# Attention and two networks on one core: one program instead of two, and another order of work where they meet

## Chip, core and metric

The kernel runs on one core of one Trainium2 chip. The metric is the time on the device in microseconds (us). Engines are named as in the profile: PE (TensorE, with PEld for its weight loads), DVE (VectorE), ACT (ScalarE), POOL (GpSimd) and SP (SyncE, which only issues transfers here).

## What is computed

Three stages, each feeding the next. First an attention over chunks of 32 tokens, then a network with a rational activation, then a network with a product of two projections:

```python
# attention: 4 batches, 8 heads, 768 tokens, 64 per head; 8 memory keys; 16 tokens left and 8 right of a chunk of 32
scores = scale * np.matmul(q_c, k_full.transpose(0, 1, 3, 2))
a = np.exp(scores - max); a = a / (sum(a) + 1e-09)
out[:, :, c_start:c_end] = np.matmul(a, v_full)
# x: 3072 tokens of 512
h = x @ w_in                                   # 512 -> 2048
g = (a0 + a1*h + a2*h^2 + a3*h^3) / (1 + |b0|*|h| + |b1|*h^2 + 1e-6)
x2 = g @ w_out                                 # 2048 -> 512
y = ((x2 @ w1) * (x2 @ w2)) @ w3 @ w_out2      # 512 -> 1024 -> 1024 -> 512
```

## The kernel before

**Precision.** Every matrix product of the networks is made of three products on PE, of a high and a low part: hi by hi, hi by lo, lo by hi. The high part is a copy to the type that PE multiplies, the low part is the difference. So a product of a 512x128 piece of weights with 512 tokens is 12 matmuls of 128x128 by 128x512. DVE, ACT and POOL make the parts.

**Two programs in a row.** `attention_and_weights` (L213) opens a block with a program for each engine, and so does `mlps` (L812, block at L856). All engines meet between the two blocks; the trace shows the meeting as L215. The first program folds w3 and w_out2 into one matrix, runs the attention tile by tile (24 tiles t = 0 to 23 of 128 tokens, 6 for a batch, `tile_step` on each engine), and splits the weights of the first network into parts. The second runs both networks over 6 blocks of 512 tokens.

**A tile of attention.** For tile t PE does `transpose_p` (L736: the probabilities are transposed, 8 matmuls), `scores` of tile t+3 (L716) and `pv` (L744). DVE does in one step (L630) the maximum of tile t+1, the sum of t, the subtraction of the maximum of t+1, and the division of t (`normalise`, L616). ACT does (L534) `copy_pT` of t, `exp` of t+2, `copy_xT` of t (from bank 6) and the issue of its store, `store_x`. Each engine works through its queue in order. In this text T(t), norm(t) and pv(t) are those steps of tile t. SP loads v for tile t+3 and one raw piece of w_in or w_out in its step t (L394).

**Weights of the first network.** There are 16 slots, one for each piece of 128 hidden units; a slot has four parts (w_in hi, lo, w_out hi, lo). POOL splits two raw pieces for a slot (`split_weights`, L176: a multiplication by ones for hi, L181, and a subtraction for lo, L184). Slots 0 to 13 are split during the first program; slots 14 and 15 lie where v and the transposed probabilities are kept, and so are split at the start of the second (4 pieces, L947 and the loop behind it).

**The join.** The first block of x is loaded back from the scratch tensor xT by SP at its step 15 (L413), together with the coefficients of the activation (L414, L416). ACT makes x_hi in tiles 18 and 19, two chunks each, behind the tile's other work (L529). DVE makes x_lo of chunks 0 and 2 behind its steps 19 and 20 (L668), POOL those of chunks 1 and 3 behind its last piece (L453). PE puts the products h of slot 0 and 1 with the first block into the two last tiles (L757). Bank 7 is the one in which q and k are turned; from tile 18 on it is free.

**The first network.** For slot m of block i, PE makes h(m) (`h_product`, L205) and, three slots later in its order, adds g(m) times w_out (`finish_g`, L1175, its matmuls at L1183). Between them ACT does `start_h` (|h|, h squared, a linear term; L978, L981, L982), DVE `make_s` (L1082), ACT `ln_exp` (L989, L992, the reciprocal), DVE `make_g` (L1099, L1102, L1106), ACT `g_his` (L997), DVE `make_p` of the next slot (L1089, L1092, which read PSUM) and `make_g_lo` (L1111). I write h(m), f(m) = finish_g of slot m, and g_lo(m), all of the first block unless said. POOL has one more piece of weights of the second network to split after every third g_lo, four in each of the first four blocks (L939, L944), and x_lo of two chunks.

PE's order in a tile of the first program, and its start in the second:

```python
            def tile_step(b, pos, last=False):
                turns = [] if last else [(b + 1, pos // 3, c) for c in TURNS[pos % 3]]
                transpose_p(b, pos)
                for n in turns[0:1]:
                    turn(*n)
                if not last or pos < 3:
                    pe.wait_ge(centred, TPB * b + pos + 2)
                    scores(*after(b, pos, 3))
                elif pos >= TPB - 2:
                    pe.wait_ge(centred, TILES)
                    pe.wait_ge(raw_split, 2 * EARLY + 4)
                    h_product(nc, pe, sh, slot_a, bank, 0, pos - (TPB - 2))
                for n in turns[1:2]:
                    turn(*n)
                pv(b, pos)
...
            start_h(0, 2)
            start_h(0, 3)
            finish_g(0, 0, first=True)
```

Of the kernel before, what the change touches and what calls it, by code (L numbers as in the profile page):

```python
# [79 lines left out]
SM_EPS = 1e-9  # L80
FOLD_TURNS = ((0, 0), (0, 0), (0, 0), (0, 2), (2, 5), (5, 8), (8, 11), (11, 14), (14, 16))
# [17 lines left out]
def build(nc, q, k, v, mem_k, mem_v, w_in, w_out, poly_a, poly_b, w1, w2, w3, w_out2, out,  # L99
          xT, x2T, bweights):  # L100
    with ExitStack() as ctx:
        base = (nc.sbuf_base + 31) // 32 * 32
        end = nc.sbuf_usable_end // 32 * 32

        ctx.enter_context(nc.sbuf_tensor("slab", [P, (end - base) // 4], F32))
        top = end // LINE * LINE
        slots = top - SLOTS * 4 * BLK * 4
        weights = nc.alloc_sbuf_tensor_at("weights", [P, SLOTS * 4 * BLK], F32R, offset=slots)
        work = base
        sh = Shared(nc, ctx, slots, Place(nc, top, end))  # L110
        banks = ctx.enter_context(nc.psum_tensor("banks", [P, 8, 512], F32))
        bank = [banks[:, i, :] for i in range(8)]
        attention_and_weights(nc, q, k, v, mem_k, mem_v, w_in, w_out, w3, w_out2, poly_a, poly_b,
                              xT, bweights, weights, slots, work, banks, bank, sh)
        mlps(nc, w1, w2, w_in, w_out, xT, x2T, bweights, out, weights, work, bank, sh)


class Place:
# [5 lines left out]
    def __call__(self, name, shape, dtype=F32):  # L124
# [6 lines left out]
        return t  # L131


class Shared:


    def __init__(self, nc, ctx, end, tail):
# [17 lines left out]
        self.ln_bias = tail("ln_bias", [P, 2])  # L155
        self.small = tail
# [40 lines left out]
def h_product(nc, pe, sh, slot, bank, i, m, chunks=range(KC)):  # L197


    for c in chunks:  # L200
# [3 lines left out]
        for n, (a, x) in enumerate(((0, sh.x_hi), (0, sh.x_lo), (1, sh.x_hi))):  # L204
            last = nc.tensor.matmul(bank[m % 4][:, :], slot[:, m, a, cols], x[:, c, :],  # L205
# [7 lines left out]
def attention_and_weights(nc, q, k, v, mem_k, mem_v, w_in, w_out, w3, w_out2, poly_a, poly_b,  # L213
                          xT, bweights, weights, base, work, banks, bank, sh):
    with ExitStack() as ctx:  # L215
        x_raw, x_hi, x_lo, coef = sh.x_raw, sh.x_hi, sh.x_lo, sh.coef
        x_loaded, coef_loaded, x_hi_ready = sh.x_loaded, sh.coef_loaded, sh.x_hi_ready
        wf_stored, xt_stored = sh.wf_stored, sh.xt_stored
        raw, raw_loaded, raw_hi_ready, raw_split = sh.raw, sh.raw_loaded, sh.raw_hi_ready, sh.raw_split
        qk_sb = sh.qk_sb  # L220

        def sem(name):
            return ctx.enter_context(nc.semaphore(name))

        def sem2(name):
            return [sem(f"{name}{i}") for i in range(2)]


        fold = Place(nc, base, base + KEPT * 4 * BLK * 4)
        wo2_raw = fold("wo2_raw", [P, JS, DM])  # L230
        wo2_hi = fold("wo2_hi", [P, JS, DM], F32R)
        wo2_lo = fold("wo2_lo", [P, JS, DM], F32R)
        w3_raw = fold("w3_raw", [P, 2, F2])
        w3t_hi = fold("w3t_hi", [P, 2, F2], F32R)
        w3t_lo = fold("w3t_lo", [P, 2, F2], F32R)
        wf = fold("wf", [P, 2, 2, DM], F32R)

        top = Place(nc, base + KEPT * 4 * BLK * 4, base + SLOTS * 4 * BLK * 4)
        v_sb = top("v_sb", [P, V_BUFS, 2, DM])
        pT = top("pT", [P, H, P])  # L240
        memk_sb = pT[0:B * MEM, 0:KC, :].rearrange("p a c -> p (a c)")

        at, small = Place(nc, work, sh.raw_at - 2 * BLK * 4), Place(nc, sh.small.at, sh.small.end)
        ident = small("ident", [P, P])
        ones = small("ones", [P, 1])
        neg_max = small("neg_max", [P, H])
        sums = small("sums", [P, H])
        rsums = small("rsums", [P, H])
        qT = at("qT", [P, 2, PAIRS, HALF])
        kT = at("kT", [P, 2, PAIRS, WINDOWS, KEYS])  # L250
        probs = at("probs", [P, 2, H, KEYS])
        memkT = at("memkT", [P, PAIRS, B * MEM])
        mask = at("mask", [P, 3, KEYS], BF16)
        chunks = at("chunks", [P, P], BF16)
        xt_sb = Place(nc, sh.raw_at - 2 * BLK * 4, sh.raw_at)("xt_sb", [P, 2, KC, P])


        ident_ready, ones_ready = sem("ident_ready"), sem("ones_ready")
        masks_ready, v_zeroed, k_zeroed = sem("masks_ready"), sem("v_zeroed"), sem("k_zeroed")
        wo2_loaded = [sem(f"wo2_loaded{n}") for n in range(JS // 2)]  # L260
        wo2_hi_ready, wo2_split = sem("wo2_hi_ready"), sem("wo2_split")
        w3_loaded = sem2("w3_loaded")
        w3_transposed = sem("w3_transposed")
        w3_hi_ready, w3_split = sem("w3_hi_ready"), sem("w3_split")
        folded, wf_hi_ready, wf_split = sem("folded"), sem("wf_hi_ready"), sem("wf_split")
        q_loaded, k_loaded, memk_loaded = sem2("q_loaded"), sem2("k_loaded"), sem("memk_loaded")
        v_loaded = [sem(f"v_loaded{u}") for u in range(V_BUFS)]
        turned, turned_copied, mem_placed = sem("turned"), sem("turned_copied"), sem("mem_placed")
        scored, maxed, centred, exped = sem("scored"), sem("maxed"), sem("centred"), sem("exped")
        summed, sum_eps, rsum_ready, normalised = sem("summed"), sem("sum_eps"), sem("rsum_ready"), sem("normalised")  # L270
        p_transposed, pT_ready = sem("p_transposed"), sem("pT_ready")
        pv_done, xt_ready = sem("pv_done"), sem("xt_ready")
# [12 lines left out]
        def v_count(b, pos):

            u = pos % V_BUFS
            return 16 * (b * V_PER_BATCH[u] + (6 if pos < V_BUFS else V_PER_BATCH[u]))

        block = ctx.enter_context(nc.Block())  # L290

        @block.sync
        def _(sp):
            def load_q(hb, g):
                b, f = hb // 2, hb % 2
                s0 = f * HALF + g * P
                sp.dma_start(qk_sb[:, f, 0, g * DM:(g + 1) * DM].rearrange("p (h d) -> p h d", h=H),
                             q[b, :, s0:s0 + P, :].rearrange("h s d -> s h d")).then_inc(q_loaded[f], 16)

            def load_k(hb, g):  # L300
                b, f = hb // 2, hb % 2
                s0 = f * HALF - LEFT + K_AT[g]
                lo, hi = max(-s0, 0), min(K_ROWS[g], S - s0)
                sp.dma_start(qk_sb[lo:hi, f, 1, g * DM:(g + 1) * DM].rearrange("p (h d) -> p h d", h=H),
                             k[b, :, s0 + lo:s0 + hi, :].rearrange("h s d -> s h d")).then_inc(k_loaded[f], 16)

            def load_qk(hb, gs):

# [24 lines left out]
            def load_w3(i):
# [949 lines left out]
```

## Time and profile before

| | us |
|---|---|
| median of 3 runs | 1122.7 (1122.17 to 1123.64) |
| the profiled execution | 1123.65 |
| its span, from the first to the last instruction | 1121.9 |
| PE busy | 1088.7 (97%) |
| DVE busy | 706.8 (63%) |
| ACT busy | 583.1 (52%) |
| POOL busy | 169.0 (15%) |
| mean granted TensorE clock | 0.988 |

Times in the rows are us from the start of the span. A row of a timeline has the start, the length, the engine, line, operation, what it writes and reads, and in brackets the idle time of the engine ahead of it with what ended it. "x2" is a merged pair. The mean clock is a share of 2.4 GHz, and 0.50 of it is 1.2 GHz. Stages: folding of w3 and attention up to 199, the first network's six blocks to 720, the second network's to the end.

### The profile page before, as it was taken

The page shows a single profiled execution, that of the slowest core. Times are in us where ns is not written, and L with a number is a line of the kernel's source. Part 1 is how long each engine was busy: PE and PEld are TensorE (multiplying, and loading weights), DVE is VectorE, ACT ScalarE, POOL GpSimd, SP SyncE. Part 2 cuts the span into 40 slices and gives each one's busy share as a digit, 9 for nine tenths or more (in the row PEclk, how much of TensorE's full clock was granted, in tenths as well). Part 3 has the DMA queues.
Part 4 walks back from the last instruction along what each step waited for, and adds up shares of the span by engine and source line. Part 5 has one row for each costly group of instructions (what it writes and reads, how often), then busy time and mean ns, then how long its engine had stood idle before and what let it go on. Part 6 is the DMA issues. An engine that isn't in the chain of part 4 may idle for free.

```text
span 1121.9 us, 16471 instructions
## 1 busy us (share of the span) xinstructions
PE 1088.7 (97%) x6292; PEld 896.0 (80%) x6292; DVE 706.8 (63%) x995; ACT 583.1 (52%) x960; POOL 169.0 (15%) x137
## 2 busy tenths in 40 slices
PE   8999987899999999999999999999999999999998
PEld 6877766687888888888888888888888888888886
DVE  5378875899999999999998998811212121111211
ACT  3457763677876876877787787521213122121311
POOL 4324542412122122121100100100000000000000
PEclk9999996899999999999999999999999999999999
DMA  9989994211211220121100146320202010020000
GB/s 308 265 210 248 275 259 123 75 57 48 84 56 47 71 69 28 56 85 46 56 37 0 37 150 221 116 76 1 75 0 75 0 37 37 0 75 0 37 1 38
DMA packets 138733, 97.65 MB, mean 87 GB/s; under 512 B 89548, under 2 KB 118220, under 8 KB 137676
## 3 DMA queue, kind: packets, MB, share of 16 engines
q1 hardware_dynamic: 126028, 90.92, 26.8%
q10 hardware_dynamic: 12672, 6.29, 1.9%
q8 instruction: 21, 0.34, 0.1%
q14 instruction: 12, 0.10, 0.0%
HBM read 65.74 MB, written 31.46 MB: 87 GB/s over the span
## 4 chain that ended last, share of the span: by engine, by line
PE 51%; DVE 25%; issue 4%; ACT 2%; ACTq 0%; DVEq 0%
PE banks L1199 23%; PE banks L1214 11%; PE banks L1183 9%; PE banks L205 8%; DVE nr L1102 5%; DVE nr L1099 5%; DVE nr L1106 4%; DVE g_lo L1111 3%; DVE sq L1082 3%; DVE poly L1089 3%; DVE poly L1092 1%; DVE x_lo L1068 1%; ACT y_sb L1004 1%; ACT habs L978 0%; ACT sq L981 0%
## 5 line engine op out<-in xcount | busy, mean ns | idle before, releaser
L1183 PE MATMUL banks<-g_hi,weights 128*128 128x512 f32 x768 | 253.4, 392 | 4.9 <-DVE g_lo L1111 4.8
L205 PE MATMUL banks<-x_hi,weights 128*128 128x512 f32 x768 | 253.6, 393 | 1.9 <-PEq L215 1.9
L1199 PE MATMUL banks<-x_hi,weights 128*128 128x512 f32 x768 | 244.2, 389 | 0.0
L1140 DVE TENSOR_TENSOR nr<-habs,banks 128x512 f32<-128x512 f32 x48 | 33.0, 688 | 256.7 <-ACT habs L1034 256.7
L1183 PEld LDWEIGHTS banks<-g_hi,weights 128*128 128x128 f32 x768 | 144.9, 189 | 37.7 <-DVE g_lo L1111 7.2
L205 PEld LDWEIGHTS banks<-x_hi,weights 128*128 128x128 f32 x768 | 145.7, 190 | 32.5 <-issue 2.0
L1199 PEld LDWEIGHTS banks<-x_hi,weights 128*128 128x128 f32 x768 | 144.1, 188 | 29.8
L1034 ACT ACTIVATE habs<-banks 128x512 f32<-128x512 f32 x48 | 28.6, 596 | 245.2 <-PE banks L1199 245.2
L205 PE MATMUL banks<-x_lo,weights 128*128 128x512 f32 x384 | 150.6, 392 | 0.0
L1183 PE MATMUL banks<-g_lo,weights 128*128 128x512 f32 x384 | 150.0, 391 | 0.0
L1199 PE MATMUL banks<-x_lo,weights 128*128 128x512 f32 x384 | 149.4, 389 | 0.0
L1214 PE MATMUL banks<-weights,g_hi 128*128 128x512 f32 x384 | 118.3, 389 | 0.1
L932 POOL TENSOR_TENSOR x_lo<-x_raw,x_hi 128x512 fp32r<-128x512 f32 x22 | 31.3, 1432 | 515.2 <-ACT x_hi L972 515.2
L997 ACT ACTIVATE g_hi<-nr 128x512 fp32r<-128x512 f32 x96 | 60.7, 632 | 91.5 <-DVE nr L1106 91.5
L1082 DVE SCALAR_TENSOR_TENSOR sq<-sq,bcoef,habs 128x512 f32<-128x512 f32 x96 | 73.1, 761 | 24.8 <-ACT sq L981 24.8
L989 ACT ACTIVATE rq<-sq,ln_bias 128x512 f32<-128x512 f32 x96 | 69.8, 727 | 31.4 <-DVE sq L1082 31.1
L205 PEld LDWEIGHTS banks<-x_lo,weights 128*128 128x128 f32 x384 | 72.8, 190 | 15.1
L1214 PEld LDWEIGHTS banks<-weights,g_hi 128*128 128x128 f32 x384 | 72.0, 188 | 15.4 <-DVE g_lo L1143 0.5
L1183 PEld LDWEIGHTS banks<-g_lo,weights 128*128 128x128 f32 x384 | 72.5, 189 | 14.7
L1199 PEld LDWEIGHTS banks<-x_lo,weights 128*128 128x128 f32 x384 | 72.1, 188 | 15.1
L1102 DVE SCALAR_TENSOR_TENSOR nr<-nr,rq 128x512 f32<-128x512 f32 x96 | 82.0, 854 | 3.3
L1099 DVE SCALAR_TENSOR_TENSOR nr<-sq,rq 128x512 f32<-128x512 f32 x96 | 80.9, 843 | 0.3 <-ACT rq L992 0.3
(83 smaller groups left out, 1544.0 us busy)
## 6 DMA issues: line engine op xcount, KB each, us to landing
x_raw<-x_transposed_dram SPq DMA_DIRECT2D x12, 1024.0 KB, 5.3
weights<-second_mlp_weights_dram SPq DMA_DIRECT2D x8, 1536.0 KB, 6.3
second_mlp_weights_dram<-split SPq DMA_DIRECT2D x16, 512.0 KB, 3.0
v_sb<-in_v SPq DMA_DIRECT2D x44, 160.0 KB
qk_sb<-in_q SPq DMA_DIRECT2D x24, 256.0 KB, 4.7
x_transposed_dram<-xt_sb ACTq DMA_DIRECT2D x24, 256.0 KB, 4.2
x_transposed_dram<-y_sb SPq DMA_DIRECT2D x6, 1024.0 KB, 4.9
out<-y_sb SPq DMA_DIRECT2D x5, 1024.0 KB, 4.2
```

Source lines behind the costliest of these rows:

```text
L205: last = nc.tensor.matmul(bank[m % 4][:, :], slot[:, m, a, cols], x[:, c, :], start=c == 0 and n == 0, stop=c == KC - 1 and n == 2)
L989: nc.scalar.activation(rq[:, u, :], sq[:, u, :], ACT.Ln, scale=2.0 ** -LN_SHIFT, bias=ln_bias[:, 0:1]).then_inc(ln_ready, 1)
L997: nc.scalar.activation(g_hi[:, m % G_BUFS, :], nr[:, m % 2, :], ACT.Copy).then_inc(g_hi_ready, 1)
L1082: nc.vector.scalar_tensor_tensor(out=sq[:, u, :], in0=sq[:, u, :], scalar=bcoef[:, 1:2], in1=habs[:, u, :], op0=ALU.mult, op1=ALU.add).the ...
L1089: nc.vector.tensor_tensor(out=poly[:, u, :], in0=poly[:, u, :], in1=h[:, :], op=ALU.mult)\
L1099: nc.vector.scalar_tensor_tensor(out=nr[:, u, :], in0=sq[:, u, :], scalar=Q_ONE, in1=rq[:, u, :], op0=ALU.add, op1=ALU.mult).then_inc(e_re ...
L1102: nc.vector.scalar_tensor_tensor(out=nr[:, u, :], in0=nr[:, u, :], scalar=-2.0, in1=rq[:, u, :], op0=ALU.add, op1=ALU.mult).then_inc(r1_re ...
L1106: nc.vector.scalar_tensor_tensor(out=nr[:, u, :], in0=poly[:, u, :], scalar=ncoef[:, 0:1], in1=nr[:, u, :], op0=ALU.add, op1=ALU.mult).the ...
L1111: nc.vector.tensor_tensor(out=g_lo[:, m % G_BUFS, :], in0=nr[:, m % 2, :], in1=f32(g_hi[:, m % G_BUFS, :]), op=ALU.subtract).then_inc(g_lo ...
L1183: last = nc.tensor.matmul(bank[4 + c][:, :], slot[:, m, a, cols], g[:, m % G_BUFS, :], start=m == 0 and n == 0, stop=m == SLOTS - 1 and n ...
L1199: last = nc.tensor.matmul(bank[2 * (j % 2) + w][:, :], bslot[:, j, 2 + 2 * w + a, cols], x[:, c, :], start=c == 0 and n == 0, stop=c == KC ...
L1214: last = nc.tensor.matmul(bank[4 + t][:, :], c[:, j % G_BUFS, cols], bslot[:, j, a, :], start=j == 0 and n == 0, stop=j == JS - 1 and n == 2)
```

## The change

The two blocks become one, so that the engines no longer meet between attention and networks. What was done around the meeting is put in another order.

- **SP**: the two coefficient loads go from step 15 to before step 0. The load of the first x goes from step 15 to step 14, and waits for q of the last half batch but one only to be turned. The stores that the second program waited for at its start are waited for later.
- **ACT**: x_hi is made right behind `copy_pT` of tiles 18 and 19, ahead of `exp` and `copy_xT`. The steps of tiles 22 and 23 are cut up and put between the first steps of the network.
- **DVE**: x_lo of chunks 0 and 2 behind steps 18 and 19; the coefficients after step 6; the softmax of tiles 22 and 23 around make_s of slot 0.
- **PE**: h(0) goes into tile 21 and writes to bank 7, h(1) and h(2) into tiles 22 and 23.
- **POOL**: its x_lo behind pieces 18 and 19 instead of behind both; the last 4 pieces, of slots 14 and 15, wait for g_lo of slots 1, 3, 5 and 7 of the first block.
- Buffers move so that none of the network's early writes meets one of the attention's that is in use (kT in two tensors, probs at another place, ones shared).

The diff's core, without the change of indentation:

```diff
@@ build
+        block = ctx.enter_context(nc.Block())
+        tail = attention_and_weights(nc, ctx, block, ...)
+        mlps(nc, ctx, block, tail, ...)
@@ attention_and_weights, sync
             load_qk(3, range(0, 2))
+        sp.dma_start(coef[:, 0:4], poly_a...).then_inc(coef_loaded, 16)
+        sp.dma_start(coef[:, 4:6], poly_b...).then_inc(coef_loaded, 16)
...
-                if t == TILES - TPB - 3:
-                    sp.wait_ge(turned, 1 + TURNED * (2 * B - 1))
+            if t == TILES - TPB - 4:
+                sp.wait_ge(turned, 1 + TURNED * (2 * B - 2) + PAIRS)
                     sp.wait_ge(xt_stored[0], 16 * 3)
                     sp.wait_ge(xt_stored[1], 16 * 3)
                     sp.dma_start(x_raw[:, :, :], xT[:, :, 0:BLK]).then_inc(x_loaded, 16)
-                    sp.dma_start(coef[:, 0:4], ...)
-                    sp.dma_start(coef[:, 4:6], ...)
@@ gpsimd                                     X_LO_AT = (18, 19)
-            for c in (1, 3):
-                ... x_lo of chunk c
+            if t in X_LO_AT:
+                x_lo_odd(1 + 2 * X_LO_AT.index(t))
@@ scalar
             def tile_step(b, pos, last=False):
                 copy_pT(b, pos)
+            if last and pos == 0:
+                act.wait_ge(x_loaded, 16)
+                act.wait_ge(turned, 1 + TURNED * (2 * B - 1))
+            if last and pos < 2:
+                x_his(range(2 * pos, 2 * pos + 2))
...
-            for pos in range(TPB):
+        for pos in range(TPB - 2):
                 tile_step(B - 1, pos, last=True)
@@ vector
-            for t in range(1, TILES):
-                tile_step(t // TPB, t % TPB, more=t < TILES - 1)
-                if t in (TILES - 5, TILES - 4):
-                    x_los(2 * (t - TILES + 5))
+        for t in range(1, TILES - 2):
+            tile_step(t // TPB, t % TPB)
+            if t in (TILES - 6, TILES - 5):
+                x_los(2 * (t - TILES + 6))
+            if t == TPB:
             coefficients()
@@ tensor
-                elif pos >= TPB - 2:
+            elif pos == 3:
+                pe.wait_ge(turned_copied, 1 + TURNED * 2 * B)
+                pe.wait_ge(raw_split, 2 * EARLY + 2)
+                h_product(nc, pe, sh, slot_a, bank[7], 0, 0)
+            else:
                     pe.wait_ge(centred, TILES)
-                    pe.wait_ge(raw_split, 2 * EARLY + 4)
-                    h_product(nc, pe, sh, slot_a, bank, 0, pos - (TPB - 2))
+                pe.wait_ge(raw_split, 2 * EARLY + 2 * (pos - 2))
+                h_product(nc, pe, sh, slot_a, bank[pos - 3], 0, pos - 3)
@@ mlps, gpsimd
-            pool.memset(ones[:, :], 1.0).then_inc(ones_ready, 1)
-            pool.wait_ge(ones_ready, 1)
+        pool.wait_ge(tail.pv_done, TILES)
             for t in range(LATE, LATE + REST):
                 m, w = sh.late(t)
+            pool.wait_ge(g_lo_ready, 2 * (t - LATE) + 2)
                 sh.split_weights(pool, weights, ones, 2 * EARLY + t, EARLY + t // 2 + 1, m, w)
@@ mlps, scalar
+        act.wait_ge(sh.coef_ready, 2)
             start_h(0, 0, first=True)
-            start_h(0, 1, first=True)
+        tail.copy_pT(B - 1, TPB - 2)
             ln_exp(0, 0)
+        start_h(0, 1, first=True)
+        tail.copy_xT(B - 1, TPB - 2)
+        tail.copy_pT(B - 1, TPB - 1)
+        tail.store_x(B - 1, TPB - 2)
             step(0, 0)
-            for u in range(2):
-                act.wait_ge(xt_stored[u], 16 * (TILES // 2 + 1))
+        tail.copy_xT(B - 1, TPB - 1)
             step(0, 1)
+        tail.store_x(B - 1, TPB - 1)
@@ mlps, vector
+        tail.softmax(B - 1, TPB - 2)
             make_s(0, 0)
-            make_p(0, 0)
+        tail.softmax(B - 1, TPB - 1, more=False)
+        make_p(0, 0, first=True)
             step(0, 0)
+        dve.wait_ge(tail.p_transposed, 2 * TILES)
             step(0, 1)
@@ mlps, tensor
-            start_h(0, 2)
             start_h(0, 3)
+        pe.wait_ge(tail.pT_ready, 2 * TILES)
+        pe.wait_ge(tail.xt_ready, TILES + 1)
             finish_g(0, 0, first=True)
```

## Rows read from the trace of the kernel before

**Rows 1.** Page: busy time of PE, its share, instructions; then weight loads, DVE, ACT, POOL.

```profile
PE 1088.7 (97%) x6292; PEld 896.0 (80%) x6292; DVE 706.8 (63%) x995; ACT 583.1 (52%) x960; POOL 169.0 (15%) x137
```

**Rows 2.** Busy time by stretch: first block; engines' busy us (instructions), clock, DMA share, GB/s.

```profile
212.00:299.50 87.50, 86.43 (x377) 70.94 (x377) 85.81 (x115) 63.06 (x102) 15.28 (x11) 0.99 0.14 46
```

**Rows 3.** Waits from 212 to 720: us in total, times, longest.

```profile
PE banks L1183 <- DVE g_lo L1111: 1.4, 3, 1.1
```

**Rows 4.** Timeline of PE: T(21), h(2) behind the meeting, f(0), f(1), f(13).

```profile
180.77 1.94 PE L740 MATMUL banks<-ident,probs 128*96 128x128 f32 x8 [3.33 <-DVE probs L626]
...
199.22 0.47 PE L205 MATMUL banks<-x_hi,weights 128*128 128x512 f32 x1 [1.93 <-PEq L215]
...
209.92 0.50 PE L1183 MATMUL banks<-g_hi,weights 128*128 128x512 f32 x1 [3.38 <-DVE g_lo L1111]
...
217.11 0.39 PE L1183 MATMUL banks<-g_hi,weights 128*128 128x512 f32 x1
...
280.94 0.50 PE L1183 MATMUL banks<-g_hi,weights 128*128 128x512 f32 x1 [1.07 <-DVE g_lo L1111]
```

**Rows 5.** Timeline of DVE, first block: g_lo(1), make_g beside a piece and without, g_lo(13).

```profile
215.82 0.68 DVE L1111 TENSOR_TENSOR g_lo<-nr,g_hi 128x512 fp32r<-128x512 f32 x1
...
237.94 1.53 DVE L1099 SCALAR_TENSOR_TENSOR nr<-sq,rq 128x512 f32<-128x512 f32 x1
239.50 1.66 DVE L1102 SCALAR_TENSOR_TENSOR nr<-nr,rq 128x512 f32<-128x512 f32 x1
...
244.51 0.68 DVE L1099 SCALAR_TENSOR_TENSOR nr<-sq,rq 128x512 f32<-128x512 f32 x1
245.23 0.69 DVE L1102 SCALAR_TENSOR_TENSOR nr<-nr,rq 128x512 f32<-128x512 f32 x1
...
249.28 0.68 DVE L1099 SCALAR_TENSOR_TENSOR nr<-sq,rq 128x512 f32<-128x512 f32 x1
...
280.20 0.69 DVE L1111 TENSOR_TENSOR g_lo<-nr,g_hi 128x512 fp32r<-128x512 f32 x1
```

**Rows 6.** Timeline of POOL: one piece, its high and its low part.

```profile
221.52 1.31 POOL L939 TENSOR_TENSOR split<-raw,ones 128x512 fp32r<-128x512 f32 x1 [9.06 <-DVE g_lo L1111]
222.90 1.62 POOL L944 TENSOR_TENSOR split<-raw,split 128x512 fp32r<-128x512 f32 x1
```

**Rows 7.** Timeline of ACT: the first step of start_h(0) and of ln_exp(0); start_h(1) lies between.

```profile
199.20 0.69 ACT L978 ACTIVATE habs<-banks,ncoef 128x512 f32<-128x512 f32 x1 [1.27 <-PEq L215]
...
202.64 0.75 ACT L989 ACTIVATE rq<-sq,ln_bias 128x512 f32<-128x512 f32 x1
```

**Rows 8.** Timeline of DVE at the attention's end: norm(18), x_lo of chunk 0, of chunk 2.

```profile
158.10 1.61 DVE L626 TENSOR_TENSOR probs<-probs,rsums 128x768 f32<-128x768 f32 x1
...
167.22 0.69 DVE L668 TENSOR_TENSOR x_lo<-x_raw,x_hi 128x512 fp32r<-128x512 f32 x1 [2.48 <-ACT x_hi L532]
...
174.37 1.51 DVE L668 TENSOR_TENSOR x_lo<-x_raw,x_hi 128x512 fp32r<-128x512 f32 x1 [2.56 <-ACT x_hi L532]
```

**Rows 9.** Timeline of ACT: copy_pT of tile 18, both halves.

```profile
161.87 1.08 ACT L495 ACTIVATE pT<-banks 96x512 f32<-96x512 f32 x2 [0.89 <-PE banks L740]
```

**Rows 10.** Timeline of SP: the raw piece of its step 14, and the load of x.

```profile
152.83 0.76 SPq L171 DMA_DIRECT2D raw_w<-in_moe_w_in  x1
...
157.60 0.62 SPq L413 DMA_DIRECT2D x_raw<-x_transposed_dram  x1
```

**Rows 11.** DMA issues from 130 to 200: count, KB, us from issue to landing.

```profile
x_raw<-x_transposed_dram SPq DMA_DIRECT2D x1, 1024.0 KB, 8.9
```

**Rows 12.** Busy time by stretch, columns as in Rows 2: attention before the x load; behind it; cold.

```profile
124.00:158.00 34.00, 30.54 (x540) 24.66 (x541) 26.41 (x40) 23.68 (x45) 16.65 (x16) 0.95 1.09 266
...
163.00:165.00 2.00, 1.36 (x34) 1.25 (x35) 1.67 (x3) 1.27 (x2) 0.48 (x1) 1.00 0.40 109
...
184.00:188.00 4.00, 4.00 (x39) 3.62 (x36) 3.51 (x10) 2.44 (x4) 0.00 (x0) 0.50 0.18 53
```

**Rows 13.** Timeline of PE: pv(19).

```profile
170.38 1.97 PE L753 MATMUL banks<-pT,v_sb 96*64 96x64 f32 x32 [3.36 <-DMA v_sb<-in_mem_v]
```

More of the change, by code:

```diff
@@ L131, in __call__ @@
         return t
+class Tail:
+    pass
 class Shared:
@@ L155, in __init__ @@
         self.ln_bias = tail("ln_bias", [P, 2])
+        self.ones = tail("ones", [P, 1])
         self.small = tail
@@ L194, in x_chunk_ready, with h_product @@
     pe.wait_ge(sh.x_lo_pool if c % 2 else sh.x_lo_dve, n * 2 + c // 2 + 1)
-def h_product(nc, pe, sh, slot, bank, i, m, chunks=range(KC)):
+def h_product(nc, pe, sh, slot, to, i, m, chunks=range(KC)):
     for c in chunks:
@@ new lines, in attention_and_weights, with sem, sem2 @@
+    x_raw, x_hi, x_lo, coef = sh.x_raw, sh.x_hi, sh.x_lo, sh.coef
+    x_loaded, coef_loaded, x_hi_ready = sh.x_loaded, sh.coef_loaded, sh.x_hi_ready
+    wf_stored, xt_stored = sh.wf_stored, sh.xt_stored
+    raw, raw_loaded, raw_hi_ready, raw_split = sh.raw, sh.raw_loaded, sh.raw_hi_ready, sh.raw_split
+    qk_sb = sh.qk_sb
+    def sem(name):
+        return ctx.enter_context(nc.semaphore(name))
+    def sem2(name):
+        return [sem(f"{name}{i}") for i in range(2)]
+    fold = Place(nc, base, base + KEPT * 4 * BLK * 4)
@@ new lines, in _, with place_mem, x_lo_odd @@
+    @block.gpsimd
+    def _(pool):
+        pool.memset(ident[:, :], 0.0).then_inc(ident_ready, 1)
+        pool.memset(ones[:, :], 1.0).then_inc(ones_ready, 1)
+        pool.wait_ge(ident_ready, 1)
+        pool.affine_select(out=ident[:, :], in_=ident[:, :], compare_op=ALU.not_equal, fill=1.0, base=0,
+                           pattern=[[-1, P]], channel_multiplier=1).then_inc(ident_ready, 1)
+        pool.memset(v_sb[:, :, :, :], 0.0).then_inc(v_zeroed, 1)
+        pool.wait_ge(ones_ready, 1)
+        def place_mem(hb):
+            b, f = hb // 2, hb % 2
+            if hb >= 2:
+                pool.wait_ge(scored, 3 * (hb - 1))
+            pool.tensor_copy(kT[f][:, :, :, CTX:KEYS], memkT[:, :, b * MEM:(b + 1) * MEM].unsqueeze(2)
+                             .broadcast_to([P, PAIRS, WINDOWS, MEM])).then_inc(mem_placed, 1)
+        def x_lo_odd(c):
+            pool.wait_ge(turned, 1 + TURNED * 2 * B)
+            pool.wait_ge(x_hi_ready, c + 1)
+            pool.tensor_tensor(out=x_lo[:, c, :], in0=x_raw[:, c, :], in1=f32(x_hi[:, c, :]),
+                               op=ALU.subtract).then_inc(sh.x_lo_pool, 1)
+        for n in range(2 * EARLY):
+            sh.split_weights(pool, weights, ones, n, n // 2 + 1, FIRST + n // 2, n % 2)
+        pool.wait_ge(turned_copied, 1)
+        place_mem(0)
+        place_mem(1)
+        pool.wait_ge(folded, JS)
+        for u in range(2):
+            pool.wait_ge(wf_stored[u], 16 * (JS // 2 + 1))
+        for t in range(LATE):
+            if t % 3 == 0 and t // 3 + 2 < 2 * B:
+                place_mem(t // 3 + 2)
+            m, w = sh.late(t)
+            sh.split_weights(pool, weights, ones, 2 * EARLY + t, EARLY + t // 2 + 1, m, w)
+            if t in X_LO_AT:
+                x_lo_odd(1 + 2 * X_LO_AT.index(t))
```

1716 lines of the change are left out of this document (840 added, 876 removed).

## The prediction

> **What bounds the kernel now.** I read the page first: PE is busy for 97% of the span, so the time can only come from the places where PE waits or is cold [rows 1]. In the first network's first block PE is busy 86.43 of 87.5 us, but DVE is busy 85.81 of them: two engines at their limit at once [rows 2]. The waits say what PE still lacks there: 1.4 us in all up to 720, on g_lo [rows 3]. So behind the first block PE alone sets the pace, and nothing of the change reaches that part. The timeline of PE gives the landmarks: T(21) starts at 180.77, PE stands 1.93 before h(2) at the meeting and 3.38 before f(0), f(1) starts at 217.11 and f(13) at 280.94, behind a wait of 1.07 for g_lo(13) [rows 4]. From f(13) on PE runs without a gap. **The end of the kernel moves by as much as f(13) moves.** That is the quantity I work out.
>
> What sets f(13)? From f(1) to f(13) PE does 12 f and 11 h, 23 products; 63.83 less the wait of 1.07 is 62.8, or 2.73 each, and 5.46 for a slot [rows 4]. DVE's step for a slot is 4.77 (244.51 to 249.28), less than PE's. But a piece of POOL beside it lengthens two of its instructions, 1.53 against 0.68 and 1.66 against 0.69: 1.82 a piece [rows 5]. From the end of g_lo(1), 216.50, to that of g_lo(13), 280.89, are 64.4; 12 steps are 57.2 and four pieces 7.3, together 64.5. So DVE is without a gap there and **DVE sets f(13)**, though PE looks the busier.
>
> **First term: when g_lo(1) is ready.** I follow the new order through the attention's end.
>
> The x load. It is issued behind the raw piece of step 14, some 153.6 instead of 157.60 [rows 10]. It took 8.9 [rows 11], so it lands by 162.5. Before it landed at 166.5 and x_hi waited for it; now ACT has copy_pT(18) until 162.95 first [rows 9]. x_hi of chunk 0 comes at 163.6, 3 us earlier than before.
>
> DVE's x_lo. It now stands behind norm(18), which ends at 159.7 [rows 8], and needs what follows from norm(18) itself: T(18), copy_pT(18), x_hi. DVE stands from 159.7 to 163.6, 3.9 us, where before it stood 2.48 one step later. Queued behind it are the softmax of tile 19 and all that follows. x_lo to 164.3, a step of softmax about 4.0 (from x_lo at 167.22 with 0.6 to the end of the next norm at 171.8 before), norm(19) ends at 168.3. The same once more for chunk 2: T(19), copy and x_hi take about 4.1, x_lo ends at 172.4. Before, DVE stood 2.56 there [rows 8], because x_hi was behind copy_xT(19) and so behind pv(19), which waited 3.36 for v [rows 13]. norm(20) ends at 176.4, and norm(21), which has to wait for T(20) in between, at 180.7. That is when it ended before (T(21) waited for it and began at 180.77 [rows 4]). So **the earlier x gives nothing at T(21)**: two waits of 4.0 replace waits of 5.0 in all and a late v. PE may be cold from the gap before T(20) and need some 2 us more for T(20), scores(23) and pv(20): T(21) at 180.8 to 183, I take 181.6.
>
> v(18) and v(19). SP now has the 1 MB before v(18). The DMA share before it is 1.09, so it is late by up to the length of the load, 4.4 us of transfer; v(18) was issued before 157.60 [rows 10] and used behind copy_pT(18), at 163 [rows 9], 5.4 later, so pv(18) is just covered. v(19) is behind the same bytes as before, less the two coefficient loads. Those leave a hole: in 163 to 165 the DMA share falls to 0.40 [rows 12]. v(19) comes up to 2 earlier and is needed only at 171. The coefficients' new place has a hole of the same size, 0 to 3 us; SP still waits for PE between its loads at that time, so I take 0.
>
> From T(21) to g_lo(1). T(21), h(0), pv(21) follow on PE: warm 1.1 + 2.7 + 1.1, cold (the clock was 0.50 in 184 to 188, where h(0) began [rows 12]) 1.9 + 5 + 2. I take 6.8: pv(21) ends at 188.4. Then ACT has no gap worth naming: copy_xT 0.6, its store 0.6, start_h(0) 1.8, copy_pT(22) 1.1, ln_exp(0) 1.5, start_h(1) 1.7, copy_xT(22) 0.6, copy_pT(23) 1.1, store 0.6, ln_exp(1) 1.5, g_hi(0) 0.6, start_h(2) 1.7, copy_xT(23) 0.6, ln_exp(2) 1.5, g_hi(1) 0.6 (two start_h take 3.44 and half an ln_exp 0.75 [rows 7]; two copies take 1.08 [rows 9], and I take half of that and some hand-over for one, for a g_hi and for the issue of a store). That is 16.1; with 1.1 of hand-overs and 0.8 from g_hi(1) to the end of g_lo(1), which DVE makes behind make_p(2), **g_lo(1) is ready at 206.4**, 10.1 before the 216.5 of now. PE (h(1) to h(3), pv, T: some 14 us warm) and DVE (two softmax ends, make_s to make_p: some 13) lie inside ACT's 18. The meeting's 1.93 and the idle start of DVE and ACT are within this sum.
>
> **Second term: POOL's last four pieces.** Now they run between 199 and 212, before g_lo(1). After the change they fall into the stretch from g_lo(1) to g_lo(13), behind g_lo 1, 3, 5 and 7, together with the four that are there already: the first of those is free to start behind g_lo(2), but POOL works in order, so it comes right behind the fourth. Eight pieces in 12 steps: 57.2 + 14.6 = 71.8 for DVE, against 64.5 now and 65.4 for PE. At full price the four new ones cost 7.3. A piece that starts right behind a g_lo meets the first two instructions of make_g and costs those 1.82; one that comes back to back with another, or when its transfer has landed, falls on other instructions, and no row shows what it costs there: from 0, if it meets only the two of make_p, which read PSUM, to 1.82. Two or three of the eight are such. I take 6.0 for the four more, nearer to the row, and keep 4 and 7.3 for the range.
>
> The Trainium skill, page "SBUF — State Buffer", section "SBUF: two separate sides", has the shared pair as an exclusive lock, "the loser fully blocks", for a DVE instruction with two SBUF inputs. The row shows less: POOL's piece takes 2.93 [rows 6] and DVE loses 1.82, since POOL waits a part of it. By the page's rule read as a loss of the whole piece the four would cost 11.7 and the kernel would lose 1.6 us; this is rival 2's far end.
>
> **The sum.** 10.1 - 6.0 = 4.1 us earlier at f(13), and so at the end. One meeting at the end of the kernel stays. The profiled run was 1123.65 with a span of 1121.9, the median 1122.7; from the median: **1118.6 us**.
>
> **The rivals.**
> 1. *The pieces hide.* If DVE isn't quite the bound in the new block (ACT's tail faster with a warm clock, g_lo(1) at 204.5, pieces at 1.0 each), the gain is 12 - 4 = 8: 1114.7. For it: the make_p overlap; against it: DVE's sum closes to 0.1 us. The ceiling, with PE as the bound from f(1) on, is 280.94 - (206.9 + 62.8) = 11.2: 1111.5.
> 2. *The pieces take it back.* Full price 7.3 and a cold start (g_lo(1) at 209) give 7.5 - 7.3 = 0.2; with 8 for the pieces 0 or a loss under 1: 1120.5 to 1123.5. For it: the sum with four pieces closes at full price [rows 5], and the clock was cold when h(0) ran [rows 12].
> 3. *Slower: v late behind x.* The load of x stands before v(18) while the DMA is at 1.09. If the ring does not catch up, pv(18) and pv(19) each wait, as pv(19) did with 3.36 [rows 13], each with a cold stretch behind it (about 3 us lost), and T(21) moves. The gain is gone when T(21) is later than 185.7, and it is slower than 0.2% from 188. Two stalls of 3.4 with two cold stretches and no hole saved put it at 191: 1128. Against it: v(18) had 4 us in hand.
> 4. *The cutting up doesn't bring f(0) forward.* The queues of ACT and DVE now hold attention and network in turn; if one waits for the other at each of these places, g_lo(1) comes only at 213 to 215, and the pieces still cost 6: 1125 to 1127. Against it: by the order above none of them waits over 1 us.
>
> **Chances.** Forecast (gain 2.3 to 6) 0.50, rival 1 0.16, rival 2 0.22, rival 3 0.07, rival 4 0.05. A measurement of this kernel can tell about 0.2%, 2.2 us, from no change. Faster by more: 0.50 + 0.16 = 0.66. Within: rival 2, 0.22. Slower by more: rivals 3 and 4, 0.12. The range takes in the forecast, rival 2 and the nearer half of rival 1 and leaves out some 0.1 on each side: 1114.2 to 1123.0.
>
> **What the profile after would show.** DVE x_lo (chunk 0 and 2) with a wait of about 3.9 each, on x_hi; T(21) between 180.8 and 183; ACT nearly without idle from pv(21) to g_hi(1); the end of g_lo(1) near 206.4 and the wait of 3.38 before f(0) gone or under 1. In the first block eight pairs of POOL instructions by g_lo(12), DVE without idle from g_lo(1) to g_lo(13), 70.5 long instead of 64.4, and PE waiting 6 to 7 us for g_lo in the block instead of 1.4. From f(13) on the same intervals as now. I would be wrong if g_lo(1) comes after 210, if pieces cost DVE less than 1 us, or if a wait for v shows at pv(18).

## The result, and the profile after

| | before | after |
|---|---|---|
| median of 6 runs, us | 1122.49 (1120.88 to 1123.74) | 1118.74 (1117.21 to 1120.27) |
| span of the profiled execution | 1121.9 | 1117.5 |

The ratio is 0.9963, with a 95% interval of 0.995 to 0.9976: some 3.7 us gained, where 4.1 were forecast. Single executions of one kernel lie up to 4 us either side of its median here, so a landmark of one trace in the attention has that much room; I come back to this. The two profiled executions, 1123.65 and 1119.28, lie 1.2 and 0.5 above their medians.

The page of the changed kernel, busy time by engine, against [rows 1]:

```profile
PE 1083.3 (97%) x6292; PEld 891.6 (80%) x6292; DVE 712.3 (64%) x995; ACT 582.6 (52%) x960; POOL 169.3 (15%) x136
```

PE is busy for 5 us less and DVE for 5.5 us more, with the same number of instructions. PE's part is in the main the clock: from T(21) to f(13) it does the same products in 86.6 instead of 93.0 us of busy time, at a granted clock of 1.00 instead of 0.78 up to g_lo(1). DVE's 5.5 can't be read as the second term alone: it is busy 5.4 more from g_lo(1) to f(13), 4.4 less from T(21) to g_lo(1), where the four pieces were before, and the rest lies in the attention, where executions differ (e11, the same kernel, has 715.9).

PE's timeline of the changed kernel, T(21), f(0), f(1) and f(13), against [rows 4]:

```profile
185.21 1.08 PE L758 MATMUL banks<-ident,probs 128*96 128x128 f32 x8 [0.59 <-DVE probs L642]
...
203.48 0.39 PE L1220 MATMUL banks<-g_hi,weights 128*128 128x512 f32 x1
...
208.92 0.39 PE L1220 MATMUL banks<-g_hi,weights 128*128 128x512 f32 x1
...
276.53 0.50 PE L1220 MATMUL banks<-g_hi,weights 128*128 128x512 f32 x1 [1.75 <-DVE g_lo L1143]
```

T(21) comes 4.4 us later than before, f(0) 6.4 earlier and without a wait, f(1) 8.2 earlier, f(13) only 4.4 earlier. The end follows f(13): 1117.5 - 276.53 = 841.0, and before it was 1121.9 - 280.94 = 841.0.

DVE's timeline of the changed kernel: x_lo of chunks 0 and 2 (against [rows 8]), then g_lo(1) and g_lo(13) (against [rows 5]):

```profile
167.83 0.87 DVE L684 TENSOR_TENSOR x_lo<-x_raw,x_hi 128x512 fp32r<-128x512 f32 x1 [5.09 <-ACT x_hi L547]
...
176.59 0.78 DVE L684 TENSOR_TENSOR x_lo<-x_raw,x_hi 128x512 fp32r<-128x512 f32 x1 [3.25 <-ACT x_hi L547]
...
206.01 0.68 DVE L1143 TENSOR_TENSOR g_lo<-nr,g_hi 128x512 fp32r<-128x512 f32 x1
...
275.79 0.68 DVE L1143 TENSOR_TENSOR g_lo<-nr,g_hi 128x512 fp32r<-128x512 f32 x1
```

From the end of g_lo(1), 206.69, to that of g_lo(13), 276.47, are 69.8 us, where it was 64.4. The waits of PE in the changed kernel from 206 to 720, against [rows 3]:

```profile
PE banks L1220 <- DVE g_lo L1143: 4.3, 6, 1.7
```

So in these two traces the changed kernel has g_lo(1) 9.8 us earlier and loses 5.4 of that in the first block, where DVE is now the bound by a wider margin.

### The profile page after: what moved, and what is told of

Same layout as the page of the kernel before. It is cut to its first block, busy times and chain, and to the rows that moved or that the text cites. A ratio compares the mean times of both kernels' runs of the same rounds, so it can differ in the third digit from the quotient of the medians.

```text
span 1117.5 us, 16467 instructions
## 1 busy us (share of the span) xinstructions
PE 1083.3 (97%) x6292; PEld 891.6 (80%) x6292; DVE 712.3 (64%) x995; ACT 582.6 (52%) x960; POOL 169.3 (15%) x136
## 4 chain that ended last, share of the span: by engine, by line
PE 60%; DVE 28%; issue 6%; ACT 4%; DMA 1%; ACTq 1%; SPq 0%; DVEq 0%
PE banks L1236 23%; PE banks L1251 11%; PE banks L1220 9%; PE banks L214 8%; DVE nr L1134 5%; DVE nr L1131 5%; PE banks L711 4%; DVE nr L1138 4%; DVE sq L1114 4%; DVE g_lo L1143 3%; DVE poly L1121 3%; PE banks L730 1%; PE banks L758 1%; DVE poly L1124 1%; DVE probs L642 1%
## 5 line engine op out<-in xcount | busy, mean ns | idle before, releaser
L957 POOL TENSOR_TENSOR x_lo<-x_raw,x_hi 128x512 fp32r<-128x512 f32 x22 | 31.3, 1431 | 515.2 <-ACT x_hi L999 515.2
L1016 ACT ACTIVATE rq<-sq,ln_bias 128x512 f32<-128x512 f32 x96 | 69.8, 727 | 31.4 <-DVE sq L1114 30.8
```

The costliest lines, as they stand in the source:

```text
L1016: nc.scalar.activation(rq[:, u, :], sq[:, u, :], ACT.Ln, scale=2.0 ** -LN_SHIFT, bias=ln_bias[:, 0:1]).then_inc(ln_ready, 1)
```

## The experiments

All times are medians. The kernel before was run again beside each group of experiments, and every ratio is to those runs: its median was 1122.1 beside e1, e2, e3 and e5, 1121.3 beside e6 to e9, and 1121.0 beside e10 to e12. A median of one group against one of another has this 1 us of room, and more: the changed kernel itself had 1118.7 and 1117.4.

| run | what | us | ratio to the kernel before |
|---|---|---|---|
| changed kernel | | 1118.7 | 0.9963 [0.995, 0.9976] |
| e11_after | the same again | 1117.4 | 0.9971 [0.9957, 0.9984] |
| e1_xlo_late | x_lo one step later | 1114.3 | 0.9941 [0.9921, 0.996] |
| e2_ungated | last four pieces at once | 1118.6 | 0.9976 [0.9963, 0.9988] |
| e3_shift | second network's pieces one block on | 1113.8 | 0.9943 [0.9927, 0.9958] |
| e5_before_spread | kernel before, pieces spread | 1123.9 | 1.0023 [1.0011, 1.0035] |
| e6_coef_late | coefficients late again | 1116.6 | 0.9958 [0.9943, 0.9974] |
| e7_xlo_shift | e1 and e3 together | 1107.7 | 0.9889 [0.9862, 0.9916] |
| e12_xlo_shift | the same again | 1109.3 | 0.9894 [0.9871, 0.9917] |
| e8_xload_15 | e1, x loaded at step 15 | 1112.7 | 0.9931 [0.9909, 0.9952] |
| e9_in_turn | one program, nothing interleaved | 1126.7 | 1.0049 [1.0032, 1.0065] |
| e10_all | e7, x and coefficients late | 1108.2 | 0.9878 [0.9854, 0.9902] |

**The pieces spread, alone (e5_before_spread).** In the kernel before:

```diff
             for t in range(LATE, LATE + REST):
                 m, w = sh.late(t)
+                pool.wait_ge(g_lo_ready, 2 * (t - LATE) + 2)
```

> The kernel before with one part of the change alone: POOL's last four pieces wait for g_lo of slots 1, 3, 5 and 7. Theory A: g_lo(1) comes 2 to 4 us earlier than 216.5, since six of DVE's instructions before it were lengthened (about 4 us in all, not all on the path), and then four more pieces in DVE's stretch cost 5.4: 1 to 3 us slower than before, 1123.5 to 1125.5. Rival B: spreading is the part that gains: 1119 to 1121.

It measured 1123.9, 1.8 us slower than the kernel before beside it, as expected. DVE's timeline of this kernel, g_lo(1) and g_lo(13):

```profile
210.77 0.68 DVE L1112 TENSOR_TENSOR g_lo<-nr,g_hi 128x512 fp32r<-128x512 f32 x1
...
280.55 0.69 DVE L1112 TENSOR_TENSOR g_lo<-nr,g_hi 128x512 fp32r<-128x512 f32 x1
```

g_lo(1) ends at 211.45, 5.05 earlier than before, and g_lo(13) at 281.24, 0.35 later: the stretch is 69.8, as in the changed kernel. In front of g_lo(1) the four pieces had cost 4.4 (T(21) to g_lo(1) is 31.3 here and was 35.7); in the first block they cost 5.4. Spreading them was no gain by itself.

**The pieces at once, in the changed kernel (e2_ungated).**

```diff
-            pool.wait_ge(g_lo_ready, 2 * (t - LATE) + 2)
```

> The changed kernel with one edit: POOL's last four pieces do not wait for g_lo of slots 1, 3, 5 and 7, they start when pv(23) is done. Theory A: DVE has no idle time between the last norm and g_lo(13), so a piece costs it the same wherever it falls; g_lo(1) comes 2 to 3 us later, the stretch behind it is shorter by as much: 1118 to 1119.5, the spreading is worth nothing. Rival B: while the first slots are filled ACT is the bound and DVE's lengthening hides: 2 to 3 us gained, about 1116.

1118.6: no change from 1118.7. It is made of two parts: from T(21) to the end of g_lo(1) this trace has 26.2 us (187.35 to 213.52) where the changed kernel has 21.5, and from there to g_lo(13) 65.4 (to 278.94) where it has 69.8. Two stretches with opposite signs, 4.7 and 4.4. The expectation had the reason slightly wrong: DVE does have idle time behind the last norm of the changed kernel, ahead of make_s(0).

```profile
192.68 0.75 DVE L1114 SCALAR_TENSOR_TENSOR sq<-sq,bcoef,habs 128x512 f32<-128x512 f32 x1 [3.62 <-ACT sq L1008]
```

But in e2 the pieces begin at 202.96, behind that place, and from there on DVE's rows have no wait. So a piece costs about the same on either side of g_lo(1).

**The second network's pieces one block later (e3_shift).** POOL's four pieces in each of the first four blocks go to blocks 1 to 4:

```diff
-        with pool.Fori(0, NBLK - 2) as i:
+        x_los(1)
+        with pool.Fori(0, NBLK - 2) as i:
             for n in range(PIECES):
-                pool.wait_ge(g_lo_ready, i * SLOTS + 3 * n + 3)
+                pool.wait_ge(g_lo_ready, (i + 1) * SLOTS + 3 * n + 3)
                 piece_hi(i, n)
                 piece_lo(i, n)
-            x_los(i + 1)
-        with pool.Fori(0, NBLK + 1) as i:
-            x_los(i + NBLK - 1)
+            x_los(i + 2)
+        with pool.Fori(0, NBLK) as i:
+            x_los(i + NBLK)
```

(SP loads and stores the pieces one block later too.)

> The changed kernel with one edit: the four pieces of the second network's weights that POOL splits in the first block, and all later ones, move one block on (blocks 1 to 4 instead of 0 to 3). Then only four pieces lie beside DVE from g_lo(1) to g_lo(13). Theory A: DVE sets f(13) and a piece costs it 1.3 to 1.8, so the stretch goes from 69.8 to 64.4, and PE becomes the bound (f(1) at 208.9 plus 62.8): f(13) at 271.8 instead of 276.5, 1114. Block 4 has DVE busy 80.3 of 87.5 and takes four pieces without loss. Rival B: the pieces' cost hides behind PE: 1118 to 1119. Rival C: block 4 loses what block 0 gains: 1118.

1113.8. The waits of PE for g_lo in this kernel, from 195 to 715, and its busy times in a stretch of g_lo(1) to g_lo(13) and in 87 us of block 4 (us, PE, PEld, DVE, ACT, POOL, clock, DMA share, GB/s):

```profile
PE banks L1227 <- DVE g_lo L1150: 0.2, 1, 0.2
```

```profile
201.80:268.20 66.40, 66.23 (x292) 54.47 (x291) 65.10 (x89) 47.69 (x76) 12.42 (x9) 1.00 0.05 13
557.50:644.50 87.00, 86.87 (x384) 71.57 (x383) 84.85 (x114) 64.36 (x104) 14.84 (x10) 1.00 0.17 58
```

4.3 us of waits became 0.2. PE is busy 66.23 of 66.40, so PE is the bound now, as the expectation had it; and block 4, with its four pieces more, still has PE busy 86.87 of 87. From g_lo(1) to g_lo(13) this trace has 64.4 us, as before the change. The price of the pieces was real, and there was a free place for four of them.

**x_lo one step later (e1_xlo_late).**

```diff
-            if t in (TILES - 6, TILES - 5):
-                x_los(2 * (t - TILES + 6))
+            if t in (TILES - 5, TILES - 4):
+                x_los(2 * (t - TILES + 5))
```

> The changed kernel with one edit: DVE makes x_lo of chunks 0 and 2 behind its steps 19 and 20, as before the change, instead of 18 and 19. Theory A (my prediction's picture): DVE stood 5.1 and 3.25 us for x_hi in the changed kernel, at a place where x_hi hangs on T and copy_pT of the same tile; one step later x_hi is there, both waits fall under 1 us, T(21) comes 5 to 6 us earlier (185.2 to about 180), and with it g_lo(1) and f(13): 1113 to 1114. Rival B: PE or the v loads set that stretch, not DVE, and the waits only move: under 1 us, 1118 to 1119.

1114.3. DVE's timeline of this kernel, both x_lo, without a wait:

```profile
166.97 1.53 DVE L684 TENSOR_TENSOR x_lo<-x_raw,x_hi 128x512 fp32r<-128x512 f32 x1
...
173.94 1.52 DVE L684 TENSOR_TENSOR x_lo<-x_raw,x_hi 128x512 fp32r<-128x512 f32 x1
```

From T(18) to T(21) it needs 16.2 us. The same interval in all traces:

| x_lo behind DVE's steps | x_hi | T(18) to T(21), us | mean |
|---|---|---|---|
| 19 and 20 | late (kernel before, e5) | 20.7, 20.6 | 20.6 |
| 18 and 19 | early (changed kernel, e2, e3, e6, e9, e11) | 20.8, 24.2, 22.6, 23.9, 23.5, 22.2 | 22.9 |
| 19 and 20 | early (e1, e7, e8, e10, e12) | 16.2, 14.0, 16.7, 19.1, 17.8 | 16.8 |

The groups don't overlap, though the first two nearly touch. **The move of x_lo on DVE by one step lost some 6 us in this interval.** This is shown, since e1 and the changed kernel, and e7 and e3, differ in nothing else: their medians lie 4.4 and 6.1 apart. The rest of the change at this place was worth some 4 us. I put that down to the early x_hi, but no run has x_hi alone put back. A rival: the kernel before and e5 have a wait of 3.4 and 3.9 at pv(19) for v, and none of the five traces of the last row has one there.

**Both together (e7_xlo_shift, e12_xlo_shift).**

> The changed kernel with both edits that gained: x_lo behind DVE's steps 19 and 20, and the second network's pieces one block later. Theory A: the two are terms of one sum, T(21) 5 to 6 us earlier and the stretch from g_lo(1) to g_lo(13) 5.4 shorter, cut off where PE is the bound, f(1) plus 62.8: 1108 to 1110. Rival B: with DVE relieved, PE was already the bound in one of them and the gains overlap: 1112 to 1114.

1107.7, and 1109.3 when run again. The gains add up: 4.4 of the one and 4.9 of the other from 1118.7 give 1109.4. By its ratio e1 alone overlaps a little with the changed kernel; that of e7, at most 0.9916, lies below those of e1 and e3, so each edit gains beside the other too. x_lo's place moves g_lo(1), the pieces' place the stretch behind it.

**One program with nothing interleaved (e9_in_turn).** ACT, DVE and PE do the last two tiles first, as before, but without the meeting:

```diff
         act.wait_ge(sh.coef_ready, 2)
+        for pos in (TPB - 2, TPB - 1):
+            tail.copy_pT(B - 1, pos)
+            tail.copy_xT(B - 1, pos)
+            tail.store_x(B - 1, pos)
         start_h(0, 0, first=True)
-        tail.copy_pT(B - 1, TPB - 2)
-        ln_exp(0, 0)
         start_h(0, 1, first=True)
...
         tail.softmax(B - 1, TPB - 2)
-        make_s(0, 0)
         tail.softmax(B - 1, TPB - 1, more=False)
+        make_s(0, 0)
...
-            elif pos == 3:
...
+            elif pos >= TPB - 2:
+                h_product(nc, pe, sh, slot_a, bank[7 if pos == TPB - 2 else 1], 0, pos - (TPB - 2))
...
+        start_h(0, 2)
         start_h(0, 3)
```

> The changed kernel without the interleaving: one program and no meeting, but ACT and DVE finish tiles 22 and 23 before the network's first step, and PE puts h(0) and h(1) in tiles 22 and 23 and h(2), h(3) behind, as before the change. It has only the meeting less than the kernel before at this place. Theory A: the meeting itself was worth about 1 us, as start_h(0) has to wait for copy_xT(23) anyway, and the gain is the interleaving: from T(21) to g_lo(1) 29 to 31 us instead of 21.5, 1125 to 1128. Rival B: the meeting was most of it: 1119 to 1121.

1126.7, 5.3 us slower than the kernel before beside it. ACT's timeline of this kernel at the join, the last copy of the attention and the first step of the network:

```profile
198.32 0.60 ACT L516 ACTIVATE xt_sb<-banks 128x512 f32<-128x512 f32 x1 [2.57 <-PE banks L771]
...
199.53 0.69 ACT L1002 ACTIVATE habs<-banks,ncoef 128x512 f32<-128x512 f32 x1 [0.62 <-ACT xt_sb L516]
```

start_h(0) begins 1.2 us behind that copy. In the kernel before it began at 199.20 [rows 7], 1.9 behind the copy:

```profile
197.34 0.60 ACT L501 ACTIVATE xt_sb<-banks 128x512 f32<-128x512 f32 x1 [2.52 <-PE banks L753]
```

So the meeting itself held ACT by 0.7. T(21) on PE and g_lo(1) on DVE in e9:

```profile
184.53 1.08 PE L758 MATMUL banks<-ident,probs 128*96 128x128 f32 x8
```

```profile
212.77 0.68 DVE L1138 TENSOR_TENSOR g_lo<-nr,g_hi 128x512 fp32r<-128x512 f32 x1
```

From T(21) to the end of g_lo(1) e9 has 28.9 us, the kernel before 35.7, e5 31.3, the changed kernel 21.5. Of the 35.7 - 21.5 = 14.2, 4.4 are the four pieces moved out (before to e5) and 2.4 the meeting with what else differs from e5 to e9. Most of these 2.4 is the clock: from T(21) to T(23), with T, h(0) and pv in it, e5 needs 10.5 at a clock of 0.54 and then 0.78, and e9 8.8 at 1.00. **7.4 are the interleaving**, in which I count that h(0) to h(2) come a tile earlier on PE. The same 21.5 stands in the traces of e1, e3, e6, e8 and e11.

That this kernel is slower than before, with a join 6.8 us shorter, fits the other parts of the change that it keeps: T(18) to T(21) is 2.8 longer (23.5), the stretch behind g_lo(1) 5.4, and T(18) comes 0.95 later. That makes f(13) 2.3 later, as the traces have it (283.27 and 280.94) and as the two profiled executions differ. The medians differ by 5.3, since 1123.65, the profiled execution of the kernel before, is 2.3 above the median of that kernel beside e9, and e9's own is 0.7 below its median.

**The places of the loads.** e8 is e1 with SP's load of x at step 15 (`if t == TILES - TPB - 3`), e6 is the changed kernel with the coefficient loads behind x's and `coefficients()` behind step 21, e10 is e7 with both.

> The kernel of e1_xlo_late with one more edit: SP loads x at its step 15 again, as before the change, instead of 14. Theory A: x then lands some 4 us later, behind copy_pT(18), and ACT, which now has x_hi ahead of exp(20) and copy_xT(18), stands for it: 1 to 3 us more than 1114.3. Rival B: the load's place does nothing, since v(18) gains what x loses: 1114 to 1115.

> The changed kernel with one edit: the two coefficient loads go back behind the load of x (now at step 14), and DVE makes the coefficients behind its step 21. Theory A: the place of these loads only moves a hole of some 2 us in the DMA traffic; v of the next tiles lands up to 2 us later, DVE's waits for x_hi cover that: within 1 us of the changed kernel, 1118 to 1120. Rival B: the hole stood on the path of the attention's end, and bringing it away was part of the gain: 1121 or more.

> The kernel of e7_xlo_shift with two more edits undone from the change: SP loads x at its step 15 again and the coefficients behind it, DVE makes them behind step 21. Each alone was 1.6 to 2 us below what it was compared with, in other calls. Theory A: those are the spread from call to call, the places of these loads are worth nothing: within 1 us of e7_xlo_shift, 1107 to 1109. Rival B: they add up: 1104 to 1105.

> The changed kernel itself once more, on the same chip as e10_all, to see what the spread from call to call is. Theory A: within 1.5 us of 1118.7. Rival B: 1116 to 1117, then e6_coef_late was no gain at all.

> The kernel of e7_xlo_shift once more, on the same chip as e10_all, so that the two can be compared. Theory A: 1107 to 1109, and e10_all within 1 us of it. Rival B: e10_all is 2 us or more below it.

e8 measured 1112.7, against 1114.3 for e1: my theory A, 1 to 3 us slower, was wrong. Its mechanism is there: ACT stands 2.11 for x, DVE's first x_lo waits 1.16, and pv(19) waits 2.40 for copy_pT(19). PE's timeline of e8:

```profile
168.20 1.42 PE L771 MATMUL banks<-pT,v_sb 96*64 96x64 f32 x32 [2.40 <-ACT pT L510]
```

But T(18) to T(21) is only 0.5 longer than in e1, and e8 has no wait for v. e6 measured 1116.6, less than the lower end of its expectation, and the changed kernel itself 1117.4 when run again, so e6 is no gain that can be told. e10 against e12 beside it: 1108.2 and 1109.3. So the places of the x load and of the coefficient loads are worth under 1.5 us, which these runs can't tell from nothing.

## Why the prediction was right, and where it was right by luck

**The end moves with f(13)**: right, and exactly. In the traces of before, changed, e1, e2, e5 and e9, whose f(13) starts at 280.94, 276.53, 270.73, 278.99, 281.30 and 283.27, the end of the span lies 840.9 to 841.0 behind it.

**DVE sets f(13)**: right. PE's waits on g_lo in the block are 4.0 us; I had said 6 to 7, because I had f(1) start about 0.5 behind g_lo(1), and it starts 2.2 behind it.

**The second term, 6.0 for four pieces more**: measured 5.4 (69.8 - 64.4). Five of the eight pieces start behind a g_lo and cost the 1.82 of [rows 5]. Three do not; they are in the changed kernel's timeline of POOL (one back to back, two when their transfer has landed) and of DVE beside the first of them:

```profile
243.93 1.49 POOL L964 TENSOR_TENSOR split<-raw,ones 128x512 fp32r<-128x512 f32 x1
245.50 1.62 POOL L969 TENSOR_TENSOR split<-raw,split 128x512 fp32r<-128x512 f32 x1
251.08 1.04 POOL L964 TENSOR_TENSOR split<-raw,ones 128x512 fp32r<-128x512 f32 x1 [3.96 <-DMA raw<-in_moe_w]
...
257.81 1.58 POOL L964 TENSOR_TENSOR split<-raw,ones 128x512 fp32r<-128x512 f32 x1 [3.96 <-DMA raw<-in_moe_w]
```

```profile
244.55 1.41 DVE L1138 SCALAR_TENSOR_TENSOR nr<-poly,ncoef,nr 128x512 f32<-128x512 f32 x1
245.89 0.68 DVE L1121 TENSOR_TENSOR poly<-poly,banks 128x512 f32<-128x512 f32 x1
246.60 0.75 DVE L1124 SCALAR_TENSOR_TENSOR poly<-poly,ncoef,banks 128x512 f32<-128x512 f32 x1
```

The high part of the first lengthens L1138 from 0.75 to 1.41; its low part runs from 245.50 to 247.12 beside the two instructions of make_p, which keep their 0.68 and 0.75. That piece cost 0.65. The second cost 1.03 and the third 1.88, by the distances of the g_lo around them (5.79 and 6.64 against 4.76). With five of 1.82 and twelve steps of 4.76 that makes 69.8, the whole stretch. Beside an instruction with an operand in PSUM the piece is free. I had written that no row shows this, but the trace before has one: POOL's L184 at 200.48 runs for 1.83 us beside L1089 and L1092, which keep their 0.69 and 0.75. The Trainium skill, page "SBUF — State Buffer", section "SBUF: two separate sides", has a DVE instruction with two SBUF inputs and a GpSimd one that reads SBUF contend for a port pair, which the first to start holds for its whole instruction while "the other fully blocks" (the words that I quoted, "the loser fully blocks", stand in the page's table of terms). The trace agrees on who meets whom. DVE loses 1.82 of a piece's 2.93, not all of it as in my 11.7, and the page has it lose only what is left of the instruction that it meets.

**The first term, g_lo(1) at 206.4**: measured 206.69, but by luck: two errors cancel. T(21) was to be at 181.6 and came at 185.21, close to the 185.7 from which on I had seen no gain at all; from T(21) to g_lo(1) were to be 24.8 and were 21.5.

Two things put T(21) too early. The first is my step on x_lo. I had the two waits on DVE as 3.9 and some 3.3 to 4; they were 5.09 and 3.25. The second lies ahead of it: in that trace T(18) was already at 164.39, 4.3 later than in the trace before, behind a wait of pv(16) for v:

```profile
155.81 1.97 PE L771 MATMUL banks<-pT,v_sb 96*64 96x64 f32 x32 [1.78 <-DMA v_sb<-in_v]
```

(PE's timeline of the changed kernel.) PE stood there from 154.03 on, and the load of x was issued at 155.16, so that load did not begin the wait. When the same kernel was run again (e11) T(18) was at 160.04 and T(21) at 182.20. I had taken T(18) to stay where it was. It is at 160.1 and 159.6 in the kernel before and e5, and by the mean at 161.7 in the six traces with x_lo behind steps 18 and 19, at 161.0 in the other five; whether the change does this, two traces of the old order can't tell. From T(18) to T(21) the change has 20.8 to 24.2 against 20.6: I had 21.5 against 20.65, and the mean of six is 22.9. So the mechanism was right and the size was small by about 1.4. By the means T(21) comes 4.1 us later with the change, where I had 0.8. The sum of the means, 14.2 of the join less 4.1 and 5.4, is 4.7, against the 3.7 of the medians.

The second interval was too long by 3.3. One part is the clock: I took T(21), h(0) and pv(21) half cold, 6.8; in this trace PE had less idle time ahead of T(21) (0.59 instead of 3.33), they ran at full clock and took 4.9. That is not the new order by itself. PE's timeline of e7:

```profile
174.00 1.94 PE L758 MATMUL banks<-ident,probs 128*96 128x128 f32 x8 [1.71 <-DVE probs L642]
```

In e7, e10 and e12 PE stood 1.7 to 3.6 ahead of T(21), the three took 6.3 to 6.4 at a mean clock of 0.73 to 0.76, and from T(21) to g_lo(1) were 22.9 to 23.1. The other part is ACT's chain: 18.0 against 16.6. I had put 1.1 us of hand-overs in, and had counted the issue of tile 22's store as ACT's time; in the rows copies go on while it is issued. ACT's timeline of the changed kernel, both halves of copy_pT(23) and the store:

```profile
197.72 0.60 ACT L510 ACTIVATE pT<-banks 96x512 f32<-96x512 f32 x1
197.88 0.54 ACTq L522 DMA_DIRECT2D x_transposed_dram<-xt_sb  x1
198.20 0.60 ACT L510 ACTIVATE pT<-banks 96x512 f32<-96x512 f32 x1
```

**The rivals.** 1 (the pieces hide) is refuted by e3: with four pieces less PE's waits vanish. 2 (they take it all back) falls with the 5.4; its far end, a loss of 1.6 us, would have been 1124.3 and not the 1123.5 that I gave. 3 (v late behind x) shows its mechanism but not its size: behind the load of x the changed kernel, e1, e2, e6 and e10 have no wait for v, and e11, e3, e7, e9 and e12 have one at pv(18), of 0.46, 1.11, 1.33, 3.12 and 3.20. The same kernel has it or not (changed kernel and e11). e8, which loads x a step later, has none and can't be told from e1. What a wait at pv(18) costs was not measured. e9 is what rival 4 would have looked like: g_lo(1) at 213.45.

**What stays open.** The spread between executions of one kernel, 3 to 7 us, is as large as most parts of the change. The traces show waits for v or k at other tiles in each (pv(14), pv(16), pv(18)), and some have a stretch at half clock behind; what decides where they fall was not tried. Most landmarks here are read from one trace of a kernel.

## What to carry to other kernels

When two stages are joined, follow the bound engine through the join and into the first steps of the next stage: what is moved out of the join to an engine that is full there is paid for again (4.4 won, 5.4 lost here), and a block further on the same work was free. An engine that queues up work which depends, through other engines, on what it has just finished stands for the whole way round. Let it do one more step of other work first: x_lo one tile later turned two waits of 3 to 5 us into none (e1). The gain of merging the two programs was in the main the interleaving it allows (7.4 us), not the meeting it saves (0.7 on ACT). With both repairs the kernel takes 1107.7 to 1109.3, 1.1% less than before.

## What the runs showed of the hardware that I had not expected

- A POOL piece of 2.93 us costs DVE between 0.65 and 1.88, by which DVE instructions it meets (changed kernel), and nothing beside those with an operand in PSUM: its low part from 245.50 to 247.12 ran beside two that kept their 0.68 and 0.75.
- T(21), h(0) and pv(21) took 4.9 us at a clock of 1.00, with PE idle 0.59 ahead of them (changed kernel), and 6.3 to 6.4 at a mean of 0.73 to 0.76, with PE idle 1.7 to 3.6 ahead (e7, e10, e12). The join was 1.5 us longer for it, which no operation count shows.
